# Linear attention, gated MLP and a routed MLP on one core: order of the work inside a pass

## What is computed

```
# attention: B, H, S, D = 4, 8, 768, 48; state S is D x D for each head
for t in range(S):
    new_re = ar * S_re - ai * S_im
    new_im = ar * S_im + ai * S_re
    S_re, S_im = new_re + outer(k[t], v[t]), new_im
    y[t] = q[t] @ S_re
# gated MLP: 3072 tokens, d_model 384, d_ff 1536
xn = x / rms(x) * rms_g
h = silu(xn @ w_gate) * (xn @ w_val)
x2 = h @ w_out
# routed MLP: the expert of the largest logit, d_ff 1024
out = gate_w * (relu(x2 @ w1[e]) @ w2[e])
```

## Time and profile before

| | us |
|---|---|
| median of 3 runs | 1305.37 (1302.71 to 1305.89) |
| the profiled execution, its own time | 1303.45 |
| its span, first to last instruction | 1301.7 |
| start to pass 0 | 34.0 |
| pass 0 | 79.3 |
| pass 1 | 70.8 |
| passes 2 to 10 | 655.1 (72.8 each; 71.2 to 74.8) |
| pass 11 | 68.6 |
| passes 12 and 13 | about 64 |
| experts | about 330 |

### The profile page before, as it was taken

One profiled execution on the slowest core, in us unless ns is written; L12 is line 12 of the kernel. 1 busy time (PEld: TensorE's weight loads), 2 busy tenths in 40 slices (PEclk: granted clock), 3 DMA queues, 4 the chain that ended last, 5 costly groups with the idle time before them and its releaser, 6 DMA issues. The chain is left out here.

```text
span 1301.7 us, 46434 instructions
## 1 busy us (share of the span) xinstructions
PE 1203.5 (92%) x20081; PEld 1041.7 (80%) x20081; DVE 766.8 (59%) x1549; ACT 600.7 (46%) x1293; POOL 366.4 (28%) x361
## 2 busy tenths in 40 slices
PE   1788999999999999999999999999978999999996
PEld 0556787879687887878687887878857999999996
DVE  5696847485767658484667557263117555555553
ACT  3646354545546554646455554434222344333442
POOL 8506051323333150413333150200003122222221
PEclk9899999999999999999999999999997999999998
DMA  7142011111202020111111020000005634333410
GB/s 206 26 123 59 7 39 40 39 40 33 45 15 57 9 58 20 38 40 39 39 30 42 9 45 10 15 15 3 13 13 161 209 127 143 132 134 131 137 37 30
DMA packets 151845, 78.36 MB, mean 60 GB/s; under 512 B 130715, under 2 KB 144571, under 8 KB 151664
## 3 DMA queue, kind: packets, MB, share of 16 engines
q1 hardware_dynamic: 143264, 59.04, 17.0%
q0 software_dynamic: 4384, 11.88, 3.1%
q10 hardware_dynamic: 4016, 4.73, 1.0%
HBM read 66.15 MB, written 11.06 MB: 59 GB/s over the span
## 5 line engine op out<-in xcount | busy, mean ns | idle before, releaser
L887 PE MATMUL pO<-wo_sb,hid 128*128 128x384 f32 x576 | 206.9, 496 | 4.0 <-issue 2.8
L572 DVE TENSOR_TENSOR hid<-silu,pGV 128x256 f32<-128x256 f32 x144 | 60.0, 417 | 177.2 <-ACT silu L711 177.2
L887 PEld LDWEIGHTS pO<-wo_sb,hid 128*128 128x128 f32 x576 | 102.6, 191 | 58.6 <-issue 5.2
L873 PE MATMUL pGV<-xT_hi,wg_hi 128*128 128x256 f32 x432 | 139.4, 323 | 6.1 <-DVE hid L572 6.1
L711 ACT ACTIVATE silu<-pGV 128x256 f32<-128x256 f32 x144 | 55.4, 385 | 181.1 <-PE pGV L875 178.9
L1198 ACT ACTIVATE h_hi<-pH 128x256 fp32r<-128x256 f32 x128 | 49.1, 385 | 164.9 <-PE pH L1143 164.9
L875 PE MATMUL pGV<-xT_hi,wg_lo 128*128 128x256 f32 x432 | 122.4, 283 | 1.0 <-issue 1.0
L874 PE MATMUL pGV<-xT_lo,wg_hi 128*128 128x256 f32 x432 | 122.0, 282 | 0.0
L873 PE MATMUL pGV<-xT_hi,wv_hi 128*128 128x256 f32 x432 | 121.5, 281 | 0.0
L874 PE MATMUL pGV<-xT_lo,wv_hi 128*128 128x256 f32 x432 | 121.5, 281 | 0.0
L875 PE MATMUL pGV<-xT_hi,wv_lo 128*128 128x256 f32 x432 | 121.2, 281 | 0.0
(11 more groups left out here) (213 smaller groups left out, 3043.9 us busy)
## 6 DMA issues: line engine op xcount, KB each, us to landing
w_sb<-in_moe_w SPq DMA_DIRECT2D x18, 1536.0 KB, 10.5
re<-in_a_re SPq DMA_DIRECT2D x24, 192.0 KB, 2.9
im<-in_a_im SPq DMA_DIRECT2D x24, 192.0 KB, 3.7
qin<-in_q SPq DMA_DIRECT2D x24, 192.0 KB, 2.8
kin<-in_k SPq DMA_DIRECT2D x24, 192.0 KB, 3.6
vin<-in_v SPq DMA_DIRECT2D x24, 192.0 KB, 3.3
routed_rows<-x ACTq DMA_DIRECT2D x24, 192.0 KB, 2.0
wo_sb<-in_moe_w_out SPq DMA_DIRECT2D x1, 2304.0 KB, 9.5
```

The costliest lines, as they stand in the source:

```text
L572: w.tensor_tensor(hid[:, f, :], act_g[f % 2], pGV[f % 2][:, TOKS:2 * TOKS], ALU.mult).then_inc(sm["h_ready"], 1)
L873: mm.matmul(to, hi, x_hi[:, kk, :], start=(kk == 0), stop=False)
L887: ins = mm.matmul(pO[:, 0:HD], hid[:, f, s_ * P:(s_ + 1) * P], wo_sb[:, f, :], start=(f == 0), stop=(f == NF - 1))
```

## The change

It moves steps in the list and does some work elsewhere; nothing that the kernel computes is different.

- **Gates**: level 0 is followed by gate 0, levels 1 to 5 by two gates each (1 and 2, ..., 9 and 10), level 6 by gate 11. Before, gates 0 to 4 stood singly behind levels 2 to 6 and gates 5 to 11 between `turn_back`, `output` and `state`.
- **Output projection**: `out` 0 to 3 get a stage of their own, `finA`, which works on pair i-1, the pair of the same pass's gates. They stand behind `turn_back` 0, `output` 1, `state` 0 and `output` 3. `out` 4 to 11 stay in `fin` (pair i-2) and stand between the turns, the last one behind level 0.
- `phase` 0 and 1 stand one level earlier (levels 4 and 5), `own` 0 and 1 and `rotate` 0 too; `rotate` 0 now stands ahead of `turn_back` 0, `rotate` 1 ahead of `turn_back` 1. `route` and `logits` stand behind levels 2 and 3.
- **Lead-in**: DVE clears `A`, ACT copies the masks (a step `masks` in pass -1), nobody waits for all constants. `wo_sb` is loaded later. The six `split` steps are spread over the turns, levels 2, 4 and 6 and behind output 1. BUSY_TURNS is 1 and BUSY_LEVELS 2: 44 such matmuls instead of 70.

The core of the diff:

```diff
-BUSY_TURNS, BUSY_LEVELS, BUSY_END = 2, 3, 1
+BUSY_TURNS, BUSY_LEVELS = 1, 2
 OUT_PARTS = 6
+OUT_FIRST = 4
...
-    ("wts", "split", 2), ("lev", "level", 3), ("pre", "angle", 0), ("glu", "gate", 1),
+    ("wts", "split", 2), ("lev", "level", 2), ("fin", "route", 0), ("glu", "gate", 3), ("glu", "gate", 4),
...
-    ("lev", "state", 0), ("glu", "gate", 8), ("sq", "squares", 0), ("sq", "squares", 1), ("glu", "gate", 9),
+    ("lev", "state", 0), ("sq", "squares", 0), ("sq", "squares", 1), ("finA", "out", 2),
...
-                    for u in range(U):
-                        done(g.memset(A[u][:, :, :], 0.0))
...
+                    for u in range(U):
+                        w.memset(A[u][:, :, :], 0.0).then_inc(sm["a_cleared"], 1)
...
+                            elif step == "masks":
+                                act.wait_ge(consts, n_consts)
+                                for j in range(NBLOCK):
+                                    rows_ = slice(j * BLOCK, (j + 1) * BLOCK)
+                                    s.activation(level_mask[rows_, :, :], wide_mask[rows_, :, j * ODD:(j + 1) * ODD], ACT.Copy).then_inc(sm["masks_ready"], 1)
+                                    s.activation(own_mask[rows_, :], ident[rows_, rows_], ACT.Copy).then_inc(sm["masks_ready"], 1)
...
-                                if "lev" in stages and "fin" not in stages and step in ("gate", "out"):
-                                    busy(BUSY_TURNS if step == "out" else BUSY_LEVELS if x < 5 else BUSY_END)
+                                if "lev" in stages and step in ("gate", "out"):
+                                    busy(BUSY_TURNS if step == "out" else BUSY_LEVELS)
...
                             elif step == "out":
+                                e = m if x < OUT_FIRST else i - 2
```

More of the change, by code:

```diff
@@ L76 @@
 A_COPIES = UPPER_COPIES + NBLOCK + 1
-BUSY_TURNS, BUSY_LEVELS, BUSY_END = 2, 3, 1
+BUSY_TURNS, BUSY_LEVELS = 1, 2
 OUT_PARTS = 6
+OUT_FIRST = 4
 STEPS = [
[L83 to L92, removed]
-    ("wts", "split", 2), ("lev", "level", 3), ("pre", "angle", 0), ("glu", "gate", 1),
[L94 to L99, removed]
-    ("lev", "state", 0), ("glu", "gate", 8), ("sq", "squares", 0), ("sq", "squares", 1), ("glu", "gate", 9),
-    ("lev", "output", 2), ("lev", "output", 3), ("glu", "gate", 10), ("sq", "abs", 0), ("sq", "abs", 1), ("glu", "gate", 11),
@@ new lines @@
+    ("glu", "norm", 0), ("pre", "roots", 0), ("pre", "roots", 1), ("lev", "turn", 0), ("lev", "turn", 1), ("fin", "out", 4), ("fin", "out", 5),
+    ("lev", "turn", 2), ("lev", "turn", 3), ("pre", "sums", 0), ("pre", "sums", 1), ("fin", "out", 6),
+    ("lev", "turn", 4), ("lev", "turn", 5), ("glu", "scale", 0), ("pre", "recip", 0), ("lev", "first", 0), ("fin", "out", 7),
+    ("lev", "turn", 6), ("lev", "turn", 7), ("wts", "split", 0), ("pre", "recip", 1), ("fin", "out", 8),
+    ("lev", "turn", 8), ("lev", "turn", 9), ("pre", "quotients", 0), ("fin", "out", 9),
@@ new lines @@
+    ("lev", "turn", 10), ("lev", "turn", 11), ("lev", "first", 1), ("pre", "quotients", 1), ("wts", "split", 1), ("fin", "out", 10), ("glu", "turn_in", 0),
+    ("fin", "square", 0), ("pre", "tangent", 0), ("pre", "tangent", 1),
+    ("lev", "level", 0), ("fin", "out", 11), ("fin", "square", 1), ("glu", "gate", 0),
+    ("lev", "level", 1), ("pre", "double", 0), ("pre", "double", 1), ("glu", "gate", 1), ("glu", "gate", 2),
+    ("wts", "split", 2), ("lev", "level", 2), ("fin", "route", 0), ("glu", "gate", 3), ("glu", "gate", 4),
@@ new lines @@
+    ("lev", "level", 3), ("pre", "angle", 0), ("fin", "logits", 0), ("glu", "gate", 5), ("glu", "gate", 6),
+    ("wts", "split", 3), ("lev", "level", 4), ("pre", "angle", 1), ("pre", "phase", 0), ("glu", "gate", 7), ("glu", "gate", 8),
+    ("lev", "level", 5), ("pre", "phase", 1), ("pre", "own", 0), ("glu", "gate", 9), ("glu", "gate", 10),
+    ("wts", "split", 4), ("lev", "level", 6), ("glu", "gate", 11), ("pre", "rotate", 0), ("pre", "own", 1),
+    ("lev", "turn_back", 0), ("pre", "rotate", 1), ("finA", "out", 0), ("lev", "turn_back", 1),
@@ L102 @@
+    ("lev", "output", 0), ("lev", "output", 1), ("finA", "out", 1), ("wts", "split", 5),
+    ("lev", "state", 0), ("sq", "squares", 0), ("sq", "squares", 1), ("finA", "out", 2),
+    ("lev", "output", 2), ("lev", "output", 3), ("sq", "abs", 0), ("sq", "abs", 1), ("finA", "out", 3),
     ("lev", "state", 1),
@@ L107 @@
 FIRST_STEPS = [("pre", step, u) for step, u in (
-    ("roots", 0), ("roots", 1), ("sums", 0), ("sums", 1), ("recip", 0), ("recip", 1),
+    ("roots", 0), ("roots", 1), ("masks", 0), ("sums", 0), ("sums", 1), ("recip", 0), ("recip", 1),
     ("quotients", 0), ("tangent", 0), ("angle", 0), ("double", 0),
@@ L226, in build @@
             n_first = 9
-            n_consts = n_first + 3 + 2 * LOW + 2 * NBLOCK
+            n_consts = n_first + 1 + 2 * LOW
             def pview(u, ell):
@@ L309, in _ @@
                             queries_and_keys(0, 1)
+                            sp.dma_start(wo_sb[:, :, :], w_out.rearrange("(f p) d -> p f d", p=P)).then_inc(sm["wo_loaded"], 16)
                         if n >= 2:
@@ L356, in _ @@
                                              pattern=[[2 * L, nb], [0, L]], channel_multiplier=-1))
[L357 to L360, removed]
                     assert step == n_consts
@@ L657, in body @@
                                 if L == SEPARATE:
+                                    act.wait_ge(sm["a_cleared"], U)
                                     for u in range(U):
```

23 lines of the change are left out of this document (11 added, 12 removed).

## The result

The changed kernel is slower: 1315.0 us (median of 13 runs, 1306.1 to 1324.3) against 1305.4 (13 runs, 1302.7 to 1310.3), a ratio of 1.0069 with a 95% interval of 1.0046 to 1.0092. The forecast was 1296 in a range of 1281 to 1311. The profiled execution has a span of 1309.5 us against 1301.7.

What follows compares the result with a forecast made beforehand. PE's own work was taken to bound passes 2 to 10, DVE pass 0. Lead-in -7, passes 2 to 9 0, passes 10 and 11 -1.5 each: -10 from 1303.45, 1293.5; median 1295.4, upward lean 1296, range 1281 to 1311.

Steps and rivals of the forecast that it cites:

- The level part: Level 0 to the end of gate 11: 41.7 us, PE's level waits for DVE gone, gaining 1.4 us a pass.
- The end of the pass: Last gate to turn 2: chain over ACT, POOL, DVE 17.7 us, PE's own work 15.1, so PE waits 2.7 a pass.
- `squares` at 1.5 and 2 us: DVE's `squares` at each pass's end run beside POOL's rotations, at 1.5 and 2 us in every pass, not only pass 0.
- Rival A: DVE gets the ports before POOL, `squares` take 2.8 us, the end gains 1.4 in eight passes: 1284 us; chance 0.22.
- The 7.3 us of 'issue': PE's waits in passes 2 to 10 that no other engine ends, 7.3 us, taken as untouched by any edit.
- those that now fall into the end are hidden by the 2.7 us: Irregular PE stops at a pass's end vanish in PE's wait there: 0.3 us a pass at most, some 2 in all.
- the experts' stretch: From the last twelve `out` steps to the end of the kernel: forecast difference 0.
- Rival B: Clock falls at every pass's end after PE's 1.4 us wait before turn 2: 15 us more, 1311; chance 0.20.
- The lead-in: Passes 0 and 1 and the setup before them: together 8.5 us less, 7 taken, bounds 4 and 9.
- rival C: The lead-in gives nothing, eaten by the lower clock and DVE's moved splits: 1303, no change that can be told; chance 0.13.
- -4.1 to the end of level 6: Pass 0, DVE: level 0 starts 1.4 us later, three splits fewer in the levels save 5.5, so 4.1 less.
- Passes 10 and 11: Pass 10 has no `squares`, 1.5 us less; pass 11 has no preparation and loses its level waits, 1.5 less.

Runs made afterwards that it cites:

- good edges: Unread short matmuls before turn 2 keep block edges alike each pass; spread over four quarters: changed kernel 1290.9 us, new order on old lead-in 1288.3, kernel before 1297.2.

## Why the prediction was wrong, step by step

1. *The level part* (41.7 us, no wait for DVE left): right, 41.69.
2. *The end of the pass* (17.7 us, PE's own 15.1, waits of 2.7 with 1.4 in front of turn 2): the end was 18.5. PE's own part was 16.9, the wait in front of turn 2 0.60, the inner ones 1.0. The chain was right, PE's own term too small by 1.8: an `out` step there takes 1.5 to 1.6 us and I had put 1.3, which is half of it; the other half is 0.1 to 0.3 us in each of the other pieces.
3. *`squares` at 1.5 and 2 us*: right in passes 1 to 9 but for 3 and 7 (in pass 0 only the first of the two was slow, 1.63 and 0.35), where the stop in output 1 let POOL finish first (0.56 and 0.35). Rival A is out. DVE's busy time in passes 2 to 10 rose from 423.87 to 456.69 us. The rule of the Trainium skill that the forecast drew on (SBUF — State Buffer, section Who interferes with whom) agrees with these rows.
4. *"The 7.3 us of 'issue' are waits that no other engine ends; no edit touches them"* and *"those that now fall into the end are hidden by the 2.7 us"*: **this is the step that failed.** The stops were not chance and no constant. The new order doubled them, from 10 to 21 and 24 us, and they fell where nothing hides them. With the stops taken out by the edges, the changed kernel is at 1290.9, on the side that was forecast. Of the 19 us between the forecast and the result this step is 10 (+8.6 instead of -1.5); the lead-in (6) is 6.4 in pass 0, and the experts' stretch, which the forecast put at nothing, 4.9. From pass 11 to the last `out` steps it came 1.9 better than forecast.
5. *Rival B*, the clock falling at every pass's end because of the wait in front of turn 2: its time (1311) came nearest, its mechanism is wrong. The falls stood behind stops of supply (200.5, 296.0, 326.8 and 589.6 us in the first trace), and none came behind a turn.
6. *The lead-in*: -7 to -9 forecast. By the traces the changed kernel gains 2.3 us until pass 2 begins (184.1 to 181.8), and the two runs with the lead-in alone are 5 and 3 us slower than the kernel before, which is worse than rival C (nothing gained, nothing lost). The edges don't explain that. By the traces the experts' stretch is about 3 us longer with the new lead-in, a cost that the sum doesn't have at all; which of the lead-in's edits makes it stays open. The term that failed in pass 0 is "-4.1 to the end of level 6". DVE did come late by the two splits in the turns (level 0 at 61.98 instead of 60.34, as forecast), but from there to 98 us it then waited 1.9 us for PE, whose clock was 0.83 of full speed in pass 0 instead of 0.91, and 1.6 for ACT's part of a split (before, 1.0 and 0.5 to 100 us). POOL's rotations began at 98.23, not at 94. And the sixth split, which the forecast did not price, stood in front of the state and of `squares`:

```profile
98.23 1.96 POOL L400 TENSOR_TENSOR qcs<-cs,qin 128x768 f32<-128x768 f32 x1 [5.28 <-ACT cs L686]
```

```profile
105.61 2.23 DVE L558 SCALAR_TENSOR_TENSOR wv_lo<-hid,gcol,wv_hi 128x1536 fp32r<-128x1536 f32 x1 [1.06 <-ACT wv_hi L696]
107.76 0.60 DVE L541 SCALAR_TENSOR_TENSOR state<-pM,goes_on,state 96x384 f32<-96x384 f32 x1
```

```profile
108.62 0.39 PE L841 MATMUL pM<-vin,A 128*32 128x48 f32 x8 [3.35 <-DVE state L541]
```

7. *Passes 10 and 11*: pass 10 gave nothing (71.2, like a smooth one), pass 11 with 12 gave 3.4 us here and 5.5 with good edges; 3 were forecast for both.

## What to carry to other kernels

Where the waits list "issue" inside a run of short matmuls, number PE's instructions and look at the remainder by the block: if it is constant, as in all 241 stops here, the kernel waits for its instructions, and any edit that adds, removes or moves instructions changes the time in ways that no chain of engines shows. Keep runs of short matmuls apart by long ones, and before judging an order of work make the instruction count of a repeated pass close to a whole number of blocks, with the edges at a good place, or compare several offsets; here that alone was worth 8 us of the kernel before, 25 of the changed one, and 40 in the other direction.

## What the runs showed of the hardware

- Instructions reach PE in blocks of 256 (16.4 KB a packet). With an edge in or behind a level or a run of outputs the stop was up to 2.4 us; with good edges none in passes 3 to 10 was over 1.0. In the eighteen traces no two packets began less than 3.1 us apart. The Trainium skill, Advanced Engine Details and Errata, section ISA Cache, gives TensorE 128 KB but only two cache lines of 256 instructions. The traces agree with the two lines: the stops ended 2.2 to 3.0 us behind the start of the last packet, and that packet had begun at most 2.3 us ahead of the stop.
- Between 100 and 950 us of the eighteen traces 64 packets began 3.0 to 7.0 us behind the preceding edge. In 18 of these cases no other DMA was in flight in between, and in 14 of the 18 PE stood still in between. Whether a wait of PE holds back the next fetch was not tried.
- 28 records of short f32 matmuls took 1.05 us when all wrote the same 32 columns of the array and 0.43 us when they took turns over four groups of 32.
- A stop of about 2 us was often, not always, followed by 3.4 us at a granted clock of 0.50 (1.2 instead of 2.4 GHz), in the eighteen traces after 34 of the 70 stops over 1.5 us. In passes 2 to 10 of two traces of the changed kernel it came four and seven times; three falls at 1.7 us are 5 us (an estimate), where these passes took 663.7 and 670.0.
